# Sliding-window attention in periods of two groups: scores of both, turns and values interleaved anew, and VectorE's two code paths joined

## The chip, the cores and the metric

The kernel runs on one core of a Trainium2 chip. The metric is the device time of one execution in microseconds (us). Engines in the profile: PE is TensorE's matmuls and PEld its weight loads, DVE is VectorE, ACT is ScalarE, POOL is GpSimd, SP is SyncE, which here issues DMAs.

## What is computed

Three stages, one after the other: attention with a window and sinks (2 batches, 8 heads, 768 positions, head width 64), a gated two-layer network, and a dense mixture of four experts. Cut to what matters:

```python
# attention: q, k, v are (2, 8, 768, 64); n_sink = 4, window = 128
scores = matmul(q, k.T) / sqrt(64)
keep = (key < n_sink) | ((0 <= query - key) & (query - key < window))
a = softmax(where(keep, scores, -1e9))
x = matmul(a, v)                      # then (1536 tokens, 512)
# first network: w_in (512, 2048), w_out (2048, 512)
h = x @ w_in
x = (h * tanh(softplus(h))) @ w_out
# four experts: w1 (4, 512, 1024), w2 (4, 1024, 512)
out = sum(p[:, e] * (relu(x @ w1[e]) @ w2[e]) for e in range(4))
```

## The kernel before

**Units and groups.** Attention goes head pair by head pair: `CT` = 4 passes `ct`, of which pass 0 is written out and passes 1 to 3 are a loop on PE and DVE (ACT's and POOL's are written out). A pass has 24 units: 2 batches x 6 query tiles of 128 x 2 heads. Four units are a group, so a pass has 6 groups (`GROUPS_A`), 24 groups in all. A window of 128 lets a query tile see two key tiles and 16 sink columns, 272 columns. The first two tiles of a batch have 128 and 256 columns; so groups 0 and 3 of a pass are short, the others full. Four passes of six groups fill about the first 80 us.

**A group's way.** PE forms scores (`scores`, L650), one PSUM bank for each unit, four banks in all (`score_bank`): unit u goes to the bank of u-4 and waits for `masked`, the count of units that DVE has masked. DVE adds the mask and takes the row minimum in one custom instruction and a read of the accumulator (`mask_unit`, L1485), into one of four slots that ACT must have emptied. ACT takes the exponential (`exponent`, L1066) and sums the rows. DVE inverts the sums of a group (`invert`, L1495 and L1498), POOL multiplies (`normalise`, L479) and, in full groups, gathers the sink columns (L494). PE turns the group (`turn`, transposes L701, the sinks L704), in two halves; ACT copies the first half out (`copy_first`, L1077) and DVE the second (`copy_second`, L1533 for the sinks, L1537). PE multiplies with the values (`values`, L731, sinks L737). When a half of a batch is summed up, ACT takes `x_hi` (L1062) and DVE `x_lo` (L1505) from the bank (`take`).

**Order.** It is written out by hand for each engine; each engine runs its instructions in this order, and semaphores tie them together. A period handles one group g: on PE scores of g, values of g-3, turn of g-2 (`TURN_LAG`, `VALUES_LAG`); on DVE the second copy of g-3, two masks, the inverse of g-1, two masks, with a take before or behind; on ACT four exponentials with the first copy of g-2 among or behind them. Some periods of ACT also carry a weight split of 128x1024 (`SPLIT_AT`), some of POOL a DMA (`ADD_AT`). After the last group the first three up-projections of the network (`start_up`) lie between the last turns and values on PE.

**The first network** runs in 6 rounds `t` of 8 steps (`STEPS`). In each step s PE forms an up-projection (L635) and, three steps late (`LAG`), a down-projection (L838). Between them lies the gate: DVE `start_gate` (L1441), `gate_lo` of s-2 (L1479), `finish_first` (L1457, L1460), `square` (L1447), `finish_second` (L1467, L1473), with ACT's exponentials between. PE waits for `mish_lo`, which `gate_lo` counts. In the fourth step of a round DVE also adds up the last round (`add_up`, L1634).

**Two paths.** A flag computed from `n_sink` and `window` decides between the path for a window and a general path. The code of DVE was all in both paths: attention and all networks, `networks()`; the path for a window branches at its end over the other to the end of the program. The inputs here take the path for a window.

## Time and profile before

| | us |
|---|---|
| median of 3 runs | 853.79 |
| lowest, highest | 853.73, 853.82 |
| the profiled execution | 853.87 |
| its span, first to last instruction | 852.0 |
| PE busy in the span | 841.8 |
| DVE, ACT, POOL busy | 605.3, 401.5, 172.2 |

The span is one execution, taken by the hardware profiler; 1.9 us of its time lie around the span. Ends of matmuls are modelled and consecutive ones overlap in the records, so a PE that is busy in all its time can still have gaps between starts. The weight load that precedes each matmul has its own rows (PEld), and their starts show the rhythm better. A row of the timeline may stand for several equal instructions (x8); the number in brackets is the idle time of the engine before it and who ended it, or "issue" where nothing that the profile shows did.

### The profile page before, as it was taken

The page shows a single profiled execution, that of the slowest core. Times are in us where ns is not written, and L with a number is a line of the kernel's source. Part 1 is how long each engine was busy: PE and PEld are TensorE (multiplying, and loading weights), DVE is VectorE, ACT ScalarE, POOL GpSimd, SP SyncE. Part 2 cuts the span into 40 slices and gives each one's busy share as a digit, 9 for nine tenths or more (in the row PEclk, how much of TensorE's full clock was granted, in tenths as well). Part 3 has the DMA queues.
Part 4 walks back from the last instruction along what each step waited for, and adds up shares of the span by engine and source line. Part 5 has one row for each costly group of instructions (what it writes and reads, how often), then busy time and mean ns, then how long its engine had stood idle before and what let it go on. Part 6 is the DMA issues. An engine that isn't in the chain of part 4 may idle for free.

```text
span 852.0 us, 13889 instructions
## 1 busy us (share of the span) xinstructions
PE 841.8 (99%) x4518; PEld 729.0 (86%) x4518; DVE 605.3 (71%) x1170; ACT 401.5 (47%) x739; POOL 172.2 (20%) x259
## 2 busy tenths in 40 slices
PE   6999999999999999999999999999999999999998
PEld 5777888888888888898999899989998998899897
DVE  7888799898888989876565565565565655656655
ACT  6999754448754549753324314314413423432310
POOL 6778200001100112222012112102202202202100
PEclk9999999999999999999999999999999999999999
DMA  7455730004830006825145135225315415403304
GB/s 257 143 164 155 158 98 1 1 0 99 202 95 0 0 0 133 164 50 117 21 100 117 34 83 117 47 70 117 62 55 117 79 38 117 98 22 65 68 1 149
DMA packets 25621, 72.69 MB, mean 85 GB/s; under 512 B 4336, under 2 KB 6512, under 8 KB 25584
## 3 DMA queue, kind: packets, MB, share of 16 engines
q0 software_dynamic: 10720, 33.82, 21.9%
q1 hardware_dynamic: 14576, 38.04, 13.3%
q10 hardware_dynamic: 288, 0.39, 0.1%
q8 instruction: 16, 0.26, 0.1%
q14 instruction: 21, 0.17, 0.1%
HBM read 35.28 MB, written 3.15 MB: 45 GB/s over the span
## 4 chain that ended last, share of the span: by engine, by line
PE 99%; DMA 0%; POOL 0%; DVE 0%; issue 0%; SPq 0%; DVEq 0%
PE banks L943 31%; PE banks L869 28%; PE banks L838 15%; PE banks L635 15%; PE banks L650 3%; PE banks L731 3%; PE banks L701 3%; PE banks L737 1%; DMA pool<-kT 0%; POOL pool L479 0%; PE banks L704 0%; PE banks L956 0%; DVE pool L1485 0%; DVE pool L1842 0%; SPq L397 0%
## 5 line engine op out<-in xcount | busy, mean ns | idle before, releaser
L1767 DVE SCALAR_TENSOR_TENSOR pool<-banks,p_norm,pool 128x512 f32<-128x512 f32 x179 | 132.8, 748 | 66.1 <-PE banks L943 64.3
L943 PE MATMUL banks<-w_hi,g_lo 128*128 128x512 f32 x382 | 149.9, 392 | 0.0
L943 PE MATMUL banks<-w_lo,g_hi 128*128 128x512 f32 x382 | 149.7, 392 | 0.0
L943 PE MATMUL banks<-w_hi,g_hi 128*128 128x512 f32 x382 | 148.6, 389 | 0.0
L1290 ACT ACTIVATE g_hi<-pool 128x384 fp32r<-128x384 f32 x96 | 50.5, 526 | 190.7 <-DVE pool L1747 139.1
L869 PE MATMUL banks<-x_hi,w_lo 128*128 128x384 f32 x256 | 86.0, 336 | 0.0
L869 PE MATMUL banks<-x_hi,w_hi 128*128 128x384 f32 x256 | 85.9, 335 | 0.0
L869 PE MATMUL banks<-x_lo,w_hi 128*128 128x384 f32 x256 | 85.7, 335 | 0.0
L943 PEld LDWEIGHTS banks<-w_hi,g_lo 128*128 128x128 f32 x382 | 71.6, 188 | 15.0
L943 PEld LDWEIGHTS banks<-w_hi,g_hi 128*128 128x128 f32 x382 | 71.7, 188 | 13.8 <-issue 0.2
L943 PEld LDWEIGHTS banks<-w_lo,g_hi 128*128 128x128 f32 x382 | 71.7, 188 | 13.8
L547 POOL DMA_DIRECT2D w_lo<-w_sum x15 | 13.1, 876 | 322.9 <-ACT w_lo L1202 322.9
L1284 ACT ACTIVATE g_hi<-banks 128x384 fp32r<-128x384 f32 x32 | 15.7, 491 | 131.2 <-PE banks L869 131.2
L838 PE MATMUL banks<-g_hi,w_hi 128*128 128x512 f32 x192 | 75.1, 391 | 0.0
L635 PE MATMUL banks<-x_hi,w_hi 128*128 128x512 f32 (+1 forms) x192 | 75.1, 391 | 0.0
L838 PE MATMUL banks<-g_lo,w_hi 128*128 128x512 f32 x192 | 74.8, 390 | 0.0
L838 PE MATMUL banks<-g_hi,w_lo 128*128 128x512 f32 x192 | 74.8, 390 | 0.0
L635 PE MATMUL banks<-x_lo,w_hi 128*128 128x512 f32 (+1 forms) x192 | 74.7, 389 | 0.0
L635 PE MATMUL banks<-x_hi,w_lo 128*128 128x512 f32 (+1 forms) x192 | 74.7, 389 | 0.0
L1754 DVE SCALAR_TENSOR_TENSOR g_lo<-pool,g_hi 128x384 fp32r<-128x384 f32 x96 | 53.6, 559 | 21.6 <-ACT g_hi L1290 17.8
L1037 ACT ACTIVATE pool<-pool,two 128x512 f32<-128x512 f32 x48 | 34.8, 725 | 72.2 <-DVE pool L1447 72.2
L1725 DVE TENSOR_TENSOR pool<-banks,pool 128x384 f32<-128x384 f32 x32 | 17.8, 557 | 52.9 <-ACT pool L1221 44.5
(151 smaller groups left out, 1774.8 us busy)
## 6 DMA issues: line engine op xcount, KB each, us to landing
w_raw<-weights SPq DMA_DIRECT2D x48, 512.0 KB, 4.3
w_lo<-w_raw POOLq DMA_DIRECT2D x48, 512.0 KB, 5.5
w_lo<-w_sum POOLq DMA_DIRECT2D x15, 384.0 KB, 4.0
pool<-v SPq DMA_DIRECT2D x8, 384.0 KB, 3.3
out<-pool SPq DMA_DIRECT2D x11, 256.0 KB, 2.0
pool<-kT SPq DMA_DIRECT2D x7, 400.0 KB, 5.1
pool<-qT SPq DMA_DIRECT2D x7, 384.0 KB, 4.4
w_lo<-pool POOLq DMA_DIRECT2D x2, 384.0 KB, 4.8
```

Of the source, the lines that this page charges most:

```text
L635: mm = pe.matmul(banks[:, 4 + f % H_RING, :], w[:, f, k * P:(k + 1) * P], x[:, k, ds(c * CHUNK, CHUNK)], start=(k == 0 and n == 0), stop=( ...
L650: mm = pe.matmul(bank[:, col:col + n], q_pair[rows, b, j * P:(j + 1) * P], k_pair[rows, b, key:key + n], start=True, stop=True)
L701: mm = pe.transpose(banks[:, TURN_BANK + n, P * (2 * h + k):P * (2 * h + k) + P], window_prob(u + h, WIDE)[:, col:col + P], ident[:, :])
L731: mm = pe.matmul(banks[D * h:D * h + D, out_bank, column], v_pair[:, b, kt, D * h:D * h + D], prob_T[:, slot, P * (2 * h + k):P * (2 * h + ...
L838: mm = pe.matmul(banks[:, i, :], w[:, f, lo:hi], g_slot(h, g), start=(f == 0 and n == 0), stop=(f == STEPS - 1 and n == 2), skip_group_che ...
L869: mm = pe.matmul(banks[:, bank, 0:HALF], w_cols(w, p2 * SLOT + at + k * P, P), x_part(lo, s, name)[:, k * HALF:(k + 1) * HALF], start=(fir ...
L943: mm = pe.matmul(banks[:, bank, :], g[:, s, f * SUP + at:f * SUP + at + P], w_cols(w, p2 * SLOT + DOWN_AT[f], DM), start=(f == 0 and n == ...
L1037: act.activation(r_buf[:, s % 2, :], n_buf[:, s % 2, :], ACT.Ln, bias=two[:, 0:1]).then_inc(l_done, 1)
L1290: act.activation(relu_of(s, f, l), source, ACT.Relu).then_inc(relu_hi, 1)
L1725: dve.tensor_tensor(c12, bank(5 + s), p1_sum, ALU.add).then_inc(sum_done, 1)
L1754: dve.scalar_tensor_tensor(out=g_lo[:, s, at], in0=source, scalar=0.0, in1=g_hi[:, s, at].bitcast(f32), op0=ALU.max, op1=ALU.subtract).the ...
L1767: dve.scalar_tensor_tensor(out=to, in0=d_bank, scalar=share, in1=to, op0=ALU.mult, op1=ALU.add)\
```

## The change

On PE the period now handles two groups, g (even) and g+1: scores of g, scores of g+1, turn of g-2, values of g-3, values of g-2, turn of g-1. ACT copies the first half of g-2 behind the exponentials of g, and of g-1 behind those of g+1; its takes move accordingly. DVE's period of two groups opens as before with the second copy of g-3, then two masks, the inverse of g-1, two masks; then the take of g-4, three masks of g+1, the second copy of g-2, the inverse of g, the last mask, the take of g-3. The inverse and the copy of an even group thus come one period of a group earlier than before.

On DVE the functions of the networks move out of `networks()`. Each path runs attention and the first `OWN_ROUNDS` = 2 rounds of the first network and then branches to a common piece `dve_rounds`, which has the other four rounds and all that follows. The branch hint at DVE's end is gone. The arithmetic, the buffers, the semaphores and the DMAs are the same; POOL and SP have the same instructions.

```diff
+OWN_ROUNDS = 2
 # PE
                 def period(ct, g, before):
                     scores(ct, g)
+                    scores(ct, g + 1)
+                    even = group_at(ct, g, TURN_LAG, before)
+                    if even:
+                        turn(*even)
                     if at := group_at(ct, g, VALUES_LAG, before):
                         values(*at)
-                    if at := group_at(ct, g, TURN_LAG, before):
+                    if even:
+                        values(*even)
+                    if at := group_at(ct, g + 1, TURN_LAG, before):
                         turn(*at)
-                for g in range(GROUPS_A):
+                for g in range(0, GROUPS_A, 2):
                     period(0, g, False)
 # ACT
                 for ct in range(CT):
                     for g in range(GROUPS_A):
-                        for u in range(4 * g, 4 * g + 4):
...
-                            exponent(window_prob(u, w), scores_w[:, u % 4, 0:w], u % 4, u)
-                            if u % 4 == (1 if g % (QT // 2) == 0 or ct * GROUPS_A + g == 2 else 3):
-                                if at := group_at(ct, g, TURN_LAG, ct > 0):
-                                    copy_first(*at)
-                        if at := group_at(ct, g, VALUES_LAG, ct > 0):
-                            take_after(*at)
+                        copied = group_at(ct, g, TURN_LAG, ct > 0)
+                        if g % 2 == 0:
+                            exponents(ct, g, range(4))
+                            if copied:
+                                copy_first(*copied)
+                        else:
+                            exponents(ct, g, range(2))
+                            if at := group_at(ct, g, VALUES_LAG + 1, ct > 0):
+                                take_after(*at)
+                            exponents(ct, g, range(2, 4))
+                            if copied:
+                                copy_first(*copied)
+                            if at := group_at(ct, g, VALUES_LAG, ct > 0):
+                                take_after(*at)
 # DVE
                 def period(ct, g, before):
-                    copied = group_at(ct, g, TURN_LAG + 1, before)
-                    ended = group_at(ct, g, VALUES_LAG + 1, before)
-                    first_half = ended is not None and ended[1] % (QT // 2) == 1
-                    if copied:
-                        copy_second(*copied)
+                    if at := group_at(ct, g, TURN_LAG + 1, before):
+                        copy_second(*at)
                     mask_scores(ct, 4 * g)
                     mask_scores(ct, 4 * g + 1)
-                    if ended and not first_half:
-                        take_after(*ended)
                     if at := group_at(ct, g, 1, before):
                         invert(at[0], 4 * at[1], 4)
                     mask_scores(ct, 4 * g + 2)
                     mask_scores(ct, 4 * g + 3)
-                    if first_half:
-                        take_after(*ended)
+                    if at := group_at(ct, g, VALUES_LAG + 1, before):
+                        take_after(*at)
+                    for u in range(4 * g + 4, 4 * g + 7):
+                        mask_scores(ct, u)
+                    if at := group_at(ct, g, TURN_LAG, before):
+                        copy_second(*at)
+                    invert(ct, 4 * g, 4)
+                    mask_scores(ct, 4 * g + 7)
+                    if at := group_at(ct, g, VALUES_LAG, before):
+                        take_after(*at)
...
             with nc.body("dve_window", valid_engines=[mybir.EngineType.DVE]):
                 window_attention()
-                leaving = networks()
-                dve.br("dve_end").branch_hint(leaving)
+                rounds(0, OWN_ROUNDS)
+                dve.br("dve_rounds")
...
-            nc.switch_bb("dve_end")
+            nc.switch_bb("dve_rounds")
+            rounds(OWN_ROUNDS, NC * MISH)
```

Two places in the order of instructions. First PE in pass 0, from the scores of group 4 on. L650/L651 are scores, L701/L702 and L704/L705 turns, L731/L732 and L737/L738 values; the semaphores that an instruction waits for stand in brackets. Before:

```order
L650 MATMUL banks<-pool 128x272 [waits masked] x4
L731 MATMUL banks<-pool 64x128 [waits first_copied,masked,sink_out,sink_zero]
L731 MATMUL banks<-pool 64x128 x3
L737 MATMUL banks<-pool 64x128 x2
L731 MATMUL banks<-pool 64x128 [waits masked,second_copied]
L731 MATMUL banks<-pool 64x128 x3
L737 MATMUL banks<-pool 64x128 x2
L701 MATMUL banks<-ident,prob_third 128x128 [waits first_copied,prob_ready]
L701 MATMUL banks<-ident,prob_third 128x128 x3
```

And now, at the same place:

```order
L651 MATMUL banks<-pool 128x272 [waits masked] x8
L702 MATMUL banks<-ident,prob_third 128x128 [waits first_copied,prob_ready]
L702 MATMUL banks<-ident,prob_third 128x128 x3
L702 MATMUL banks<-ident,prob_third 128x128 [waits second_copied,prob_ready]
L702 MATMUL banks<-ident,prob_third 128x128 x2
L702 MATMUL banks<-ident,prob_third 128x128 [waits sink_out,sinks_ready]
L705 MATMUL banks<-ident,pool 64x128
L732 MATMUL banks<-pool 64x128 [waits first_copied,masked,sink_out,sink_zero]
L732 MATMUL banks<-pool 64x128 x3
L738 MATMUL banks<-pool 64x128 x2
```

Eight units' scores stand in a row where four stood, each waiting for a mask, and the turn of group 2 has moved ahead of the values of group 1.

Second, DVE in pass 0 from the second copy of group 1 on (L1553 the sinks, L1557 the rest) to the fourth mask of group 4; a mask is two rows of L1505, the inverse is L1515 and L1518. Now:

```order
L1553 COPY pool<-banks 64x128 [waits turned]
L1557 COPY pool<-banks 128x512
L1505 ISA pool,row_min<-banks,mask 128x272 [waits scored,exp_done]
L1505 ISA row_min 128x1
L1505 ISA pool,row_min<-banks,mask 128x272 [waits scored,exp_done]
L1505 ISA row_min 128x1
L1515 TENSOR_SCALAR row_den<-row_sum 128x4 [waits prob_ready,exp_done]
L1518 RECIPROCAL row_den<-row_den 128x4 [waits den_sum]
L1505 ISA pool,row_min<-banks,mask 128x272 [waits scored,exp_done]
L1505 ISA row_min 128x1
L1505 ISA pool,row_min<-banks,mask 128x272 [waits scored,exp_done]
L1505 ISA row_min 128x1
```

The twelve rows of before are the same but for the line numbers (L1533, L1537, L1485, L1495, L1498). Nothing moved here; what moved are PE's next scores, which now wait for these masks directly.

## Rows read from the trace of the kernel before

**Rows 1.** The page: busy time of each engine; PE and its clock in 40 slices.

```profile
PE 841.8 (99%) x4518; PEld 729.0 (86%) x4518; DVE 605.3 (71%) x1170; ACT 401.5 (47%) x739; POOL 172.2 (20%) x259
...
PE   6999999999999999999999999999999999999998
...
PEclk9999999999999999999999999999999999999999
```

**Rows 2.** About one attention pass: stretch, length, busy PE, PEld, DVE, ACT, POOL, clock.

```profile
35.00:55.00 20.00, 20.00 (x220) 15.47 (x220) 17.37 (x76) 18.50 (x62) 15.72 (x30) 1.00 0.56 156
```

**Rows 3.** PE's weight loads, three groups: start us, us, what, count, [idle before].

```profile
41.89 0.52 PEld L650 LDWEIGHTS banks<-pool 64*128 64x128 f32 x8 [0.17 <-issue]
42.75 0.63 PEld L731 LDWEIGHTS banks<-pool 128*64 128x64 f32 x12 [0.33 <-ACT pool L1077]
43.55 0.86 PEld L701 LDWEIGHTS banks<-ident,pool 128*128 128x128 f32 x8 [0.17 <-issue]
...
44.69 0.76 PEld L650 LDWEIGHTS banks<-pool 64*128 64x128 f32 x8 [0.20 <-DVE row_min L1485]
45.80 0.42 PEld L731 LDWEIGHTS banks<-pool 128*64 128x64 f32 x8 [0.36 <-issue]
...
47.27 0.85 PEld L701 LDWEIGHTS banks<-ident,prob_third 128*128 128x128 f32 x8 [0.17 <-issue]
...
48.40 0.76 PEld L650 LDWEIGHTS banks<-pool 64*128 64x128 f32 x8 [0.20 <-issue]
49.52 0.42 PEld L731 LDWEIGHTS banks<-pool 128*64 128x64 f32 x8 [0.36 <-issue]
...
50.98 0.64 PEld L701 LDWEIGHTS banks<-ident,pool 128*128 128x128 f32 x6 [0.17 <-issue]
51.78 0.52 PEld L650 LDWEIGHTS banks<-pool 64*128 64x128 f32 x8 [0.17 <-issue]
```

**Rows 4.** PE's weight loads at the first values behind an up-projection.

```profile
84.19 0.63 PEld L731 LDWEIGHTS banks<-pool 128*64 128x64 f32 x12 [0.35 <-issue]
```

**Rows 5.** DVE from the copy of a turned group to its fourth mask.

```profile
48.51 0.28 DVE L1533 COPY pool<-banks 64x128 f32<-64x128 f32 x1 [0.75 <-PE banks L704]
...
49.34 0.44 DVE L1485 CUSTOM_DVE_ANT_0 pool<-banks,mask 128x272 f32<-128x272 f32 x1
...
50.55 0.44 DVE L1485 CUSTOM_DVE_ANT_0 pool<-banks,mask 128x272 f32<-128x272 f32 x1
...
51.28 0.08 DVE L1485 DVE_READ_ACCUMULATOR2_ANT row_min<- 128x1 f32 x1
```

**Rows 6.** DVE in the same place, behind a short group.

```profile
51.92 0.68 DVE L1537 COPY pool<-banks 128x512 f32<-128x512 f32 x1
...
53.11 0.42 DVE L1505 TENSOR_TENSOR x_lo<-banks,x_hi 128x256 f32 x1
53.45 0.16 DVE L1495 TENSOR_SCALAR row_den<-row_sum 128x4 f32<-128x4 f32 x1
...
54.62 0.08 DVE L1485 DVE_READ_ACCUMULATOR2_ANT row_min<- 128x1 f32 x1
```

**Rows 7.** POOL, one full group.

```profile
50.53 2.44 POOL L479 TENSOR_TENSOR pool<-pool,row_den 128x272 f32<-128x272 f32 x4 [1.70 <-DVE row_den L1498]
```

**Rows 8.** The first pass: DVE's mask 11 is read; PE's scores of group 4 begin.

```profile
12.28 0.08 DVE L1485 DVE_READ_ACCUMULATOR2_ANT row_min<- 128x1 f32 x1
...
14.98 0.76 PEld L650 LDWEIGHTS banks<-pool 64*128 64x128 f32 x8 [0.20 <-issue]
```

**Rows 9.** Network, step 16: DVE's start_gate and g_lo; PE's next down-projection.

```profile
169.73 0.69 DVE L1441 TENSOR_SCALAR pool<-banks 128x512 f32<-128x512 f32 x1 [0.89 <-PE banks L635]
170.34 0.68 DVE L1479 TENSOR_TENSOR g_lo<-pool,g_hi 128x512 fp32r<-128x512 f32 x1
...
174.97 0.39 PE L838 MATMUL banks<-g_hi,w_hi 128*128 128x512 f32 x1
```

**Rows 10.** The view of DMA issues: KB each, us to landing.

```profile
prm<-params SPq DMA_DIRECT2D x1, 2.0 KB, 3.6
```

More of the change, by code:

```diff
@@ L1682, in networks, with rounds @@
+            def rounds(first, behind):
+                for t in range(first, behind):
                     for f in range(STEPS):
@@ L1757, in evict @@
-                def evict(it, s, e, first, k):
-                    dve.wait_ge(tile_done, SUP_TILES * it + k + 1)
-                    tile = TILE_ORDER[k]
-                    to, d_bank = out_acc(s, tile), banks[:, (2 * s + k) % 4, :]
-                    token = s * SUP_TILES + tile
-                    share = p_norm[:, ds(e, 1), token:token + 1].rearrange("p a n -> p (a n)")
-                    if first:
-                        dve.tensor_scalar(to, d_bank, share, None, ALU.mult).then_inc(evicted, 1)
-                    else:
-                        dve.scalar_tensor_tensor(out=to, in0=d_bank, scalar=share, in1=to, op0=ALU.mult, op1=ALU.add)\
-                           .then_inc(evicted, 1)
@@ new lines, in halves_used, with sum_16, sum_15 @@
+            def halves_used(it, n):
+                if not isinstance(it, int) or it >= 1:
+                    dve.wait_ge(relu_lo, 4 * it - 4 + n)
+            def sum_16(it, s):
+                halves_used(it, 3)
+                dve.wait_ge(prod_done, 7 * it + (3 if isinstance(it, int) and it == 0 else 2))
+                dve.wait_ge(p1_copied, it + 1)
+                dve.tensor_tensor(c12, bank(5 + s), p1_sum, ALU.add).then_inc(sum_done, 1)
+            def sum_15(it, s):
+                halves_used(it, 2)
+                if isinstance(it, int) and it == 0:
+                    dve.wait_ge(x_added[0]["T3"], 16)
+                dve.wait_ge(prod_done, 7 * it + (4 if isinstance(it, int) and it == 0 else 3))
+                dve.tensor_tensor(c22, bank(7), p1_sum, ALU.add).then_inc(sum_done, 1)
@@ new lines, in relu_rest, with evict @@
+            def relu_rest(it, s, n):
+                f, l, source = ((0, 0, bank(4)), (1, 1, c22), (0, 1, c12), (1, 0, c21))[n]
+                dve.wait_ge(relu_hi, 4 * it + n + 1)
+                at = slice(f * SUP + l * HALF, f * SUP + (l + 1) * HALF)
+                dve.scalar_tensor_tensor(out=g_lo[:, s, at], in0=source, scalar=0.0, in1=g_hi[:, s, at].bitcast(f32),
+                                         op0=ALU.max, op1=ALU.subtract).then_inc(relu_lo, 1)
+            def evict(it, s, e, first, k):
+                dve.wait_ge(tile_done, SUP_TILES * it + k + 1)
+                tile = TILE_ORDER[k]
+                to, d_bank = out_acc(s, tile), banks[:, (2 * s + k) % 4, :]
+                token = s * SUP_TILES + tile
+                share = p_norm[:, ds(e, 1), token:token + 1].rearrange("p a n -> p (a n)")
+                if first:
+                    dve.tensor_scalar(to, d_bank, share, None, ALU.mult).then_inc(evicted, 1)
+                else:
+                    dve.scalar_tensor_tensor(out=to, in0=d_bank, scalar=share, in1=to, op0=ALU.mult, op1=ALU.add)\
+                       .then_inc(evicted, 1)
@@ new lines, in _ @@
+            last = NC * MISH - 1
+            sum_16(0, 0)
+            difference(0, "T4")
+            gate_lo(NC * MISH * STEPS - 1)
+            sum_15(0, 0)
+            sum_22(0, 0)
+            sum_12(0, 0)
+            x_lo_of(0, "T4")
+            relu_rest(0, 0, 0)
+            relu_rest(0, 0, 1)
+            relu_rest(0, 0, 2)
+            dve.wait_ge(last_down, 1)
+            add_one(last, NC - 1, 0)
+            dve.wait_ge(last_down, 2)
+            add_one(last, NC - 1, 1)
+            dve.wait_ge(last_down, 3)
@@ new lines, in _ @@
+            add_one(last, NC - 1, 2)
+            dve.wait_ge(down_done, STEPS * (last + 1))
+            add_one(last, NC - 1, 3)
+            sum_21(0, 0)
+            x_lo_of(1, "B11")
+            relu_rest(0, 0, 3)
+            difference(1, "T1")
+            difference(1, "T2")
+            difference(1, "T3")
+            difference(1, "T4")
+            x_lo_of(1, "T2")
+            x_lo_of(1, "T1")
+            sum_16(1, 1)
+            x_lo_of(1, "T3")
+            sum_15(1, 1)
+            x_lo_of(1, "T4")
@@ new lines, in _ @@
+            pair_step(2 * PAIRS - 1, 1, E - 1, False)
+            for k in range(SUP_TILES - 1):
+                evict(2 * PAIRS - 1, 1, E - 1, False, k)
+            k, tile = SUP_TILES - 1, TILE_ORDER[SUP_TILES - 1]
+            for part in range(2):
+                dve.wait_ge(tile_done, SUP_TILES * (2 * PAIRS - 1) + k + part + 1)
+                to = out_acc(1, tile)[:, part * (DM // 2):(part + 1) * (DM // 2)]
+                dve.scalar_tensor_tensor(out=to, in0=banks[:, (2 + k + part) % 4, 0:DM // 2],
+                                         scalar=p_norm[:, E - 1, SUP_TILES + tile:SUP_TILES + tile + 1],
+                                         in1=to, op0=ALU.mult, op1=ALU.add).then_inc(evicted, 1)
```

260 lines of the change are left out of this document (99 added, 161 removed).

## The prediction

> **What bounds the kernel now.** I read the page first. TensorE (PE) is busy 841.8 of 852.0 us and granted full clock in all slices [rows 1]: whatever lengthens or shortens PE's own sequence moves the end by as much. In the attention stage (about 10 to 90 us) PE has no free time in the stretches of 20 us, while VectorE (DVE) has 17.37, ScalarE (ACT) 18.50 and GpSimd (POOL) 15.72 us of work in 20 [rows 2]. So I next took the timeline of PE's weight loads over three groups. It repeats with exactly 9.89 us per three groups (41.89 to 51.78), and gives each phase from start to start [rows 3]: scores (S) 0.86 us for a batch's first ("short") group and 1.12 for a full one; turns (T) 0.80 short, 1.13 full; values (V) 0.80 short, 1.46 full. In order: S .86, V .80, T 1.14, S 1.11, V 1.47, T 1.13, S 1.12, V 1.46, T .80.
>
> **What a switch costs.** A full V has 24 matmuls and takes 0.66 us more than a short one with 12, so 12 matmuls cost 0.66 and 0.14 us of the short phase is the change to the next kind of work. A full S streams 8 x 272 = 2176 columns, a short one 1536, for 0.26 us more: 0.41 ns a column, so 0.88 and 0.62 us of work and 0.24 us of switch. The loads of T are 0.11 us apart (0.86 for 8, 0.64 for 6): 0.66 of 0.80 is work, 0.14 switch. PE thus pays six switches in two groups, about 1.0 us.
>
> **Part 1, fewer switches (a gain).** Two groups now run S S T V V T. A switch after S (0.24) and one of 0.14 go away; what remains is S to T, T to V, V to T, T to S. S to T is costed like S to V (0.24, it ends the same matmuls), T to V like T to S (0.14 and up to 0.20). The trace has few of these two; the nearest worse row is the pause of 0.35 us before V after up-projections [rows 4], against 0.17 before T in the usual place. Upper bound: both 0.15 dearer. Gain taken: 0.38 us a pair, at least 0.1.
>
> In the Trainium skill, "TensorEngine Tiling (Array Packing)", section Key Properties, a change of tiling mode drains TensorE. The phases here do differ in tile shape, and the pauses agree; that page speaks for the change and has no word on what the new order waits for.
>
> **Part 2, a new wait (a loss).** Scores of unit u go to the bank that unit u-4 leaves, so they wait for the mask of u-4. Before, those masks belonged to the previous group and lay behind V and T. Now the scores of group g+1 follow at once on those of g and wait for the four masks of g. What stands ahead of these masks on DVE? Its period still opens with the second copy of the last turn, and that turn is still the last thing PE does before its scores. DVE's order up to the fourth mask is the same as now, and the trace shows how long it takes: PE starts scores at 48.40 [rows 3]; the copy starts at 48.51, the first mask at 49.34, the third (with the inverse of the sums ahead of it) at 50.55, and the last row minimum is read at 51.28 and lasts 0.08 [rows 5]. That is 2.96 us after PE's start, DVE without a pause. Adding 0.07 for the semaphore (ACT follows a mask by 0.1 us), the eighth unit's scores start 3.03 us into the period. Unhindered they would start after seven units' streaming. In pairs:
> - Groups 4,5 (both full): 2 x 0.88 less the last unit's 0.22, 1.54 us. Stall 3.03 - 1.54 = 1.49.
> - Groups 2,3 (full, short): 0.88 + 0.62 - 0.21 = 1.29. Stall 1.74.
> - Groups 0,1 (short, full): 0.62 + 0.66 = 1.28. Here the copy has no sinks and the masks are small. PE starts at 51.78, the fourth minimum is read at 54.62 plus 0.08, which is 2.92; a take of 0.34 (53.11 to 53.45) stands between and moves behind the masks, and 0.08 was a pause: 2.5, so the unit starts at 2.57 [rows 6]. Stall 1.29.
> Less 0.38 a pair, the three pairs are +1.11, +1.36 and +0.91: **+3.38 us for each pass over six groups**.
>
> Does anything else end later than PE in the stretched period? I laid one pair (4,5) out from PE's start. T of the even group starts at 3.03 + 0.22 + 0.24 = 3.49, its turn is out 1.24 later (4.7), the two copies on DVE take 0.9 (5.6). V of the odd group before it (1.32) runs from 4.6 to 5.9, then V of the even group, whose second half needs that copy only at 6.6: margin 1.0. In pair 0,1 the same margin is 0.2, the smallest. ACT's first copy waits for half the turn (4.2) and is done at 4.7. POOL needs 2.44 us for a group [rows 7]; the odd group's inverse is out at 2.15, so it is ready at 4.6 and turned at 7.4; the even group's starts at 6.0 and is needed in the next pair only, six us later. ACT's work is 18.5 in 20, or 6.1 us a pair with weight splits, under the new 7.4 to 8.2. So these cost nothing, covered by PE's own longer period; with that cover gone (were the stall not there) ACT would have only 0.1 us a pair to spare.
>
> **Part 3, the first pass.** Its scores for groups 0 to 3 now all come ahead of the first turn. The last of them waits for mask 11, whose minimum is read at 12.28 plus 0.08 [rows 8]. Then T(0) from 12.43 + 0.21 + 0.24 = 12.9, 0.80; its second copy (0.65) is out at about 14.4; V(0) 0.80, T(1) 1.13: scores of group 4 at about 16.4 instead of 14.98 [rows 8], +1.4. Pair 4,5 adds 1.11. The other pass bodies, three of them, add 3 x 3.38 = 10.1. The end (start-up of the network between the last turns) keeps its order.
>
> **Part 4, DVE's joined code.** DVE now jumps over the general path's code after round 1, between steps 15 and 16, at about 168.8 us. It waits 0.89 us for PE there anyway; the g_lo that follows it ends at 171.02 and PE uses it at 174.97 [rows 9], so another 3.9 us are free: 4.8 in all. Bounds: nothing, or one small transfer from memory, for which the 2 KB of parameters (3.6 us to landing) is the nearest [rows 10]. Either is hidden, and DVE regains 0.89 us a step. Taken: 0. The smaller program changes nothing that PE waits for.
>
> **The sum.** 1.4 + 1.1 + 10.1 = 12.6 us on the profiled execution's 853.87 (852.0 of span and 1.9 around it): 866.5, or **866.4 us** from the median 853.79. PE is full after attention, so nothing gives it back. The span should be 864.6.
>
> **The rivals.**
> - *The stall is hidden (the other side, faster).* If the masks of g were done before PE wants their banks, only the switches would remain: 11 pairs x 0.38 = 4.2 us, **849.6 us**. It decides when DVE's chain from the turn to the fourth mask is under 1.54 us. It is 2.96 by a row and has no pause in it. Only if DVE's copy came after the masks could this be; the order says otherwise. Chance 0.04.
> - *Dearer switches, or a second wait.* Both new switches at the upper bound add 0.3 us in each of 11 pairs, 3.3 in all; the small margin of pair 0,1 lost by 0.3 us adds 0.9 in three passes: **870.6 us**. The pause of 0.35 speaks for it, the pauses of 0.17 and 0.20 after T against it. Chance 0.12.
> - *Shorter stalls.* Masks on DVE that wait for nothing could move a little closer and the first pass may lose nothing: 1.4 less at the start and 0.2 less a pair, **862.8 us**. Chance 0.12.
> - *The jump of DVE.* If it took 3 us more than the 4.8 that are free, PE would stop for 3: **869.4 us**. Chance 0.03. The Trainium skill, "Runtime: NRT & Kernel Launch", section Instruction fetch mechanics, says that a taken branch out of the fetched pages stalls until its target page has been fetched. No row of this trace shows such a jump; by the page the jump costs something, and by rows it would have to cost more than 4.8 us to be seen.
> - *The change does nothing that shows:* gain and stall equal. This needs stalls of 0.4 us, a quarter of those worked out. Chance 0.02.
>
> **How the numbers follow.** The forecast's own case has 0.67. The range 861.5 to 871 takes in the rivals at 862.8, 869.4 and 870.6 and leaves out the two that end near or under the old time and what a lower granted clock would do (PE would be idle for a fifth of each pair; in the first slice of the page it is busy in only six tenths, and the granted clock is full there [rows 1], so I give that little). A measurement of this kernel can tell about 0.2% from no change. Faster 0.04, same 0.02, slower 0.94.
>
> **What would show it.** In the attention stage PE's busy share falls, with waits of S on DVE's row minimum (four units of each pair, about 1.4 us together); the pass takes 23.2 us instead of 19.8; PE's work is unchanged; the pause before V no longer stands after each S; behind attention every stretch is as long as before, shifted by 12.6 us. DVE's first instruction of step 16 may come late, with PE undisturbed. The prediction is wrong if S runs through without such waits, if PE waits on copies or POOL instead, or if the network stage gets longer.

## The result and the profile after

The changed kernel takes **867.96 us** (median; 867.81 to 869.23), the kernel before 853.82 beside it: 1.0169 times as long, 95% interval 1.0158 to 1.018. The profiled execution is itself at 867.96, 866.0 of it span. Its mean granted clock is 1.000, as in the other two of the five executions at the low end (867.81 and 867.85); the remaining two have 0.998 and took 868.77 and 869.23. The forecast was 866.4 us in 861.5 to 871.

The page of the kernel after: busy time of each engine, and PE and its clock in 40 slices.

```profile
PE 852.7 (98%) x4518; PEld 735.8 (85%) x4518; DVE 606.1 (70%) x1170; ACT 403.9 (47%) x739; POOL 172.0 (20%) x259
...
PE   7999999999999999999999999999999999999998
...
PEclk9999999999999999999999999999999999999999
```

Against [rows 1] the number of matmuls is the same, the clock is full in this execution, and only the first slices can tell anything. (PE's busy time grew by 10.9 us with the same work and the same clock. Its ends are modelled, so its share hides most of the waits; the starts of the weight loads are the better measure.) The windows of the attention stage are more distinct: stretch, length, then busy PE, PEld, DVE, ACT, POOL, and the clock.

```profile
35.00:55.00 20.00, 19.03 (x193) 14.60 (x195) 15.09 (x66) 16.21 (x54) 13.64 (x27) 1.00 0.54 154
```

In the same 20 us PE loaded weights 195 times where before it did so 220 times [rows 2], and every other engine did less too: the stage as a whole runs slower, no engine replaced PE as the one that is full. The view of waits names what PE waited for (us in total, times, longest):

```profile
PEld banks L651 <- DVE row_min L1505: 13.0, 21, 0.7
```

Before, the same wait was 1.2 us in six places of 0.2. Its place is in the timeline of PE's weight loads, here pair 4,5 of one pass: start us, us, what, count, [idle before].

```profile
40.21 0.76 PEld L651 LDWEIGHTS banks<-pool 64*128 64x128 f32 x8 [0.20 <-issue]
41.66 0.66 PEld L651 LDWEIGHTS banks<-pool 64*128 64x128 f32 x4 [0.69 <-DVE row_min L1505]
42.88 0.66 PEld L651 LDWEIGHTS banks<-pool 64*128 64x128 f32 x4 [0.56 <-DVE row_min L1505]
43.89 0.86 PEld L702 LDWEIGHTS banks<-ident,prob_third 128*128 128x128 f32 x8 [0.36 <-issue]
44.71 0.11 PEld L705 LDWEIGHTS banks<-ident,pool 128*64 128x64 f32 x1
45.02 0.42 PEld L732 LDWEIGHTS banks<-pool 128*64 128x64 f32 x8 [0.20 <-issue]
...
47.79 0.64 PEld L702 LDWEIGHTS banks<-ident,pool 128*128 128x128 f32 x6 [0.17 <-POOL pool L480]
48.60 0.52 PEld L651 LDWEIGHTS banks<-pool 64*128 64x128 f32 x8 [0.17 <-issue]
```

The first four units of scores run through, the next two pairs of units each wait for a row minimum, and turns begin 3.68 us after the scores (43.89 less 40.21). Nothing waits behind that: values follow the turn after 0.20, two groups of values run in one piece, the second turn follows after 0.17. DVE in the same stretch:

```profile
40.53 0.67 DVE L1557 COPY pool<-banks 128x512 f32<-128x512 f32 x1
41.16 0.44 DVE L1505 CUSTOM_DVE_ANT_0 pool<-banks,mask 128x272 f32<-128x272 f32 x1
41.53 0.08 DVE L1505 DVE_READ_ACCUMULATOR2_ANT row_min<- 128x1 f32 x1
...
41.89 0.17 DVE L1515 TENSOR_SCALAR row_den<-row_sum 128x4 f32<-128x4 f32 x1
...
42.37 0.44 DVE L1505 CUSTOM_DVE_ANT_0 pool<-banks,mask 128x272 f32<-128x272 f32 x1
...
43.10 0.08 DVE L1505 DVE_READ_ACCUMULATOR2_ANT row_min<- 128x1 f32 x1
```

This is the chain of [rows 5], now with PE at its end: the fourth minimum is read 2.97 us after PE began (43.10 + 0.08 less 40.21).

Starts of scores give the books of the stage. A pass over six groups lasts 19.8 us before and 23.94 after (24.66 to 48.60): pair 0,1 went from 6.51 to 7.85, pair 2,3 from 6.18 to 7.70, pair 4,5 from 7.09 to 8.39. The first pass body of the loop begins at 24.66 instead of 22.08, so the first pass lost 2.6 us. With 3 x 4.15 = 12.4 that is 15.0, and the first up-projection, the one behind the last scores, starts 15.0 us later (96.3 instead of 81.3). The network and the experts keep that distance to the last tile (861.8 instead of 846.7). Yet the span is only 14.0 us longer. One microsecond came back behind the last matmul.

### The profile page after: what moved, and what is told of

Same layout as the page of the kernel before. It is cut to its first block, busy times and chain, and to the rows that moved or that the text cites. A ratio compares the mean times of both kernels' runs of the same rounds, so it can differ in the third digit from the quotient of the medians.

```text
span 866.0 us, 13888 instructions
## 1 busy us (share of the span) xinstructions
PE 852.7 (98%) x4518; PEld 735.8 (85%) x4518; DVE 606.1 (70%) x1170; ACT 403.9 (47%) x739; POOL 172.0 (20%) x259
## 4 chain that ended last, share of the span: by engine, by line
PE 96%; DVE 1%; issue 1%; ACT 1%; DMA 0%; DVEq 0%; ACTq 0%
PE banks L951 30%; PE banks L877 27%; PE banks L846 15%; PE banks L636 15%; PE banks L702 3%; PE banks L651 2%; PE banks L732 2%; PE banks L738 1%; ACT pool L1074 1%; DVE pool L1557 0%; DMA prm<-params 0%; DVE row_min L1505 0%; PE banks L705 0%; PE banks L964 0%; DVE pool L1505 0%
```

## The experiments

### The two halves of the change

**e1**: only attention changed, in the code of before.

```diff
 def period(ct, g, before):
     scores(ct, g)
-    if at := group_at(ct, g, VALUES_LAG, before): values(*at)
-    if at := group_at(ct, g, TURN_LAG, before): turn(*at)
+    scores(ct, g + 1)
+    ... # turn(even), values(odd before), values(even), turn(odd), as in the change; ACT and DVE too
```

> Only the order of attention is changed, VectorE's two paths stay apart. Theory (the whole loss is the stall of the odd group's scores behind the even group's masks): 868 us, as the changed kernel, within 0.4. Rival (the joined code and its jump, before which the trace shows 2.27 us of idle VectorE instead of 0.89, carry part of the loss): 1.4 us less, 866.6.

Measured: 868.84 us (868.64 to 871.62), 1.0186 times before (1.0168 to 1.0203). Against the 853.86 us of before measured beside it, attention alone costs **15.0 us**, about 1 us more than the whole change. The longest of its four executions, 871.62 us, has a mean clock of 0.996; the three others have 1.000 and took 868.64 to 868.88.

**e2**: only DVE's code joined, attention in the old order.

```diff
 with nc.body("dve_window"):
     window_attention()
-    leaving = networks()
-    dve.br("dve_end").branch_hint(leaving)
+    rounds(0, OWN_ROUNDS)
+    dve.br("dve_rounds")
+# dve_rounds: rounds 2 and 3, the gate's end and the experts, once for both paths
```

> The opposite half: attention in the old order, VectorE's paths joined behind round 1. Theory: 853.8 us, no change, with a pause of about 2.3 us on VectorE ahead of step 16 and PE without a gap. Rival (the jump reaches PE): 855.2 or more, with a gap of PE in the down-projection some 5 us behind the jump.

Measured: 852.86 us (852.72 to 853.13 in ten runs), 0.9989 times before (0.9979 to 0.9998). The join is not free of effect: it **saves 1.0 us**, and makes this the fastest of all kernels here. The jump itself is in the timeline of DVE at step 16:

```profile
168.01 0.69 DVE L1474 SCALAR_TENSOR_TENSOR pool<-banks,pool 128x512 f32<-128x512 f32 x1
170.83 0.69 DVE L1442 TENSOR_SCALAR pool<-banks 128x512 f32<-128x512 f32 x1 [2.13 <-issue]
```

DVE has 2.13 us without work, against the 0.89 that it usually waits for PE [rows 9]; in the changed kernel the pause at the same step is 2.27. PE's row has no gap there in either kernel: the 4.8 us that were free cover it. By the Trainium skill, "Runtime: NRT & Kernel Launch", section Instruction fetch mechanics, a taken branch out of the fetched pages stalls until its target page is there. The trace agrees, and prices it here at 1.2 to 1.4 us more than the wait it replaces.

So where does the microsecond come from? The other jump. Before, DVE leaves the window path at the end of the program and jumps over the general path's code to the common end. The view of one source line (line, queue, operation, count, duration in ns, start) and that of waits, kernel before:

```profile
L116 SPq COMPARE_BRANCH  x1: 38/38/38, 851.3 to 851.3; - x1
...
L116 DVEq DRAIN  x1: 70/70/70, 851.7 to 851.7; - x1
...
SPq L116 <- DMA out<-pool: 2.1, 1, 2.1
```

and e2:

```profile
L117 DVEq DRAIN  x1: 524/524/524, 848.2 to 848.2; - x1
L117 SPq COMPARE_BRANCH  x1: 38/38/38, 850.5 to 850.5; - x1
...
SPq L117 <- DMA out<-pool: 1.4, 1, 1.4
```

DVE's last result is out at 848.82 before and at 848.68 in e2. Before, DVE reaches its closing drain 2.9 us later, at 851.7, behind even SP's wait for the last output; in e2 it is there at once. SP's wait for the last transfer ends 2.5 us after DVE's last result before, and 1.8 in e2; from that to the end of the span it is 0.7 against 0.4. Together 1.0 us. The second part ends with DVE's late drain. That the first, a slower last transfer, has to do with the fetching of DVE's code beside it is an inference; what the runs show is that the two go together (also in e1, with the jump: 2.5 and 3.2 us from the last result to SP's branch and to the end; and in e3, e4, e6 and e9, without it, DVE's drain starts with its last result and the end comes 2.1 to 2.2 us behind it).

### DVE's order inside the chain

**e3**: the inverse of the sums behind the four masks instead of between them.

```diff
     mask_scores(ct, 4 * g + 1)
-    if at := group_at(ct, g, 1, before): invert(at[0], 4 * at[1], 4)
     mask_scores(ct, 4 * g + 2)
     mask_scores(ct, 4 * g + 3)
+    if at := group_at(ct, g, 1, before): invert(at[0], 4 * at[1], 4)
```

> The changed kernel, but VectorE inverts the sums of the group before behind the fourth mask instead of between the second and third. It takes 0.48 us of the chain from the turn to the fourth mask. Theory (this chain paces PE): 11 pairs x 0.48 = 5.3 us less, 862.7 us, PE's wait ahead of the seventh unit's scores shorter by as much. Rival (PE is paced by what GpSimd normalises, which now starts 0.75 us later): no gain or slower, 868 to 870.

Measured: 862.68 us (862.47 to 862.82), 1.0103 times before (1.0086 to 1.012): 5.3 us less than the changed kernel. PE's loads in pair 4,5, the same place as above, and the view of waits:

```profile
38.23 0.76 PEld L651 LDWEIGHTS banks<-pool 64*128 64x128 f32 x8 [0.20 <-issue]
39.69 1.38 PEld L651 LDWEIGHTS banks<-pool 64*128 64x128 f32 x8 [0.69 <-DVE row_min L1505]
41.42 0.86 PEld L702 LDWEIGHTS banks<-ident,prob_third 128*128 128x128 f32 x8 [0.36 <-issue]
...
46.13 0.52 PEld L651 LDWEIGHTS banks<-pool 64*128 64x128 f32 x8 [0.17 <-issue]
...
PEld banks L651 <- DVE row_min L1505: 7.3, 13, 0.7
```

The second wait (0.56) is gone, the first stands as it was. Turns begin 3.19 us after the scores instead of 3.68: 0.49, the two instructions of the inverse. The pass is 22.54 us (23.59 to 46.13), 1.40 less, and the first pass gives the rest: the loop begins at 23.59 instead of 24.66.

**e4**: the copy of the turned probabilities behind the four masks too, the longest thing ahead of them.

```diff
-    if at := group_at(ct, g, TURN_LAG + 1, before): copy_second(*at)
     mask_scores(ct, 4 * g) ... mask_scores(ct, 4 * g + 3)
+    if at := group_at(ct, g, TURN_LAG + 1, before): copy_second(*at)
+    if at := group_at(ct, g, 1, before): invert(at[0], 4 * at[1], 4)
```

> The changed kernel, but VectorE makes the four masks of the even group first and the copy of the last turn and the inverse behind them. The masks can start 0.4 us after PE's first scores, so the fourth is read at 0.4 + 4 x 0.36 + 0.1 = 1.9 us instead of 2.96. Theory: 11 pairs x 1.05 = 11.6 us less, 856.4 us, a little above the kernel before. Rival (a second wait: PE's values wait for the copy, which is now out 2.8 us into the period): less than half of that gain, 862 or more.

Measured: 864.98 us (864.82 to 865.09), 1.013 times before (1.0113 to 1.0147). This was the miss that taught most. The time lies where the rival put it (862 or more), but the theory's first half failed too, not only its overlap: the kernel is slower than e3, and nothing of the copy's 0.9 us came back in the stall. DVE's first masks of pair 4,5, PE's loads around them, and one wait from the view of waits:

```profile
40.10 0.44 DVE L1505 CUSTOM_DVE_ANT_0 pool<-banks,mask 128x272 f32<-128x272 f32 x1 [1.56 <-PE banks L651]
...
37.43 0.42 PEld L732 LDWEIGHTS banks<-pool 128*64 128x64 f32 x8 [0.60 <-DVE pool L1557]
...
39.15 0.76 PEld L651 LDWEIGHTS banks<-pool 64*128 64x128 f32 x8 [0.20 <-issue]
40.60 1.38 PEld L651 LDWEIGHTS banks<-pool 64*128 64x128 f32 x8 [0.69 <-DVE row_min L1505]
...
PEld banks L732 <- DVE pool L1557: 1.7, 4, 0.6
```

DVE now stands idle for 1.56 us with the mask at the head of its queue, and still starts it 0.95 us after PE's first score (40.10 less 39.15). With the copy ahead it was also 0.95 (41.16 less 40.21). So the first score of a full group needs 0.95 us from the start of its loads until DVE begins on it, and the copy had been lying inside that time at no cost. Put behind the masks it only comes late for the values, in pair 2,3 of each looped pass (0.60, 0.37 and 0.37 us). The passes are 0.89, 0.69 and 0.69 us longer than e3's, 2.3 in all; what those waits leave of it was not taken apart.

**e7**: the other direction, one more piece of DVE's work (a take of 0.68 us) ahead of the four masks.

```diff
     if at := group_at(ct, g, TURN_LAG + 1, before): copy_second(*at)
+    if at := group_at(ct, g, VALUES_LAG + 1, before): take_after(*at)
     mask_scores(ct, 4 * g)
     ...
-    if at := group_at(ct, g, VALUES_LAG + 1, before): take_after(*at)
```

> The changed kernel, but VectorE's take of group g-4 stands ahead of the four masks instead of behind them: 0.61 us more in the chain in pair 2,3 and 0.34 us in pair 0,1 of each looped pass, none in pair 4,5. Theory (any work ahead of the fourth mask lengthens PE's period one for one): 3 x 0.95 = 2.9 us more, 870.9. Rival (the wait is set by when scores arrive, and VectorE has room): no change, 868.0.

Measured: 871.8 and 872.0 in two executions, 876.0 in two others, 1.0227 times before (1.0202 to 1.0252). The granted clock is 0.998 over the first two and 0.992 over the others; the four microseconds between them I put down to the clock, though only an execution of the longer kind was profiled. In it all of the lowered clock lies in the attention stage. Pair 2,3 in two passes: stretch, length, busy PE, PEld, DVE, ACT, POOL, clock.

```profile
61.00:65.00 4.00, 2.83 (x20) 1.87 (x19) 3.09 (x12) 2.38 (x7) 1.33 (x4) 1.00 0.00 0
65.00:71.00 6.00, 6.00 (x51) 5.09 (x52) 3.02 (x14) 4.35 (x15) 4.65 (x9) 0.72 0.04 5
...
91.00:96.00 5.00, 4.86 (x54) 4.01 (x55) 3.29 (x16) 4.49 (x17) 4.07 (x8) 1.00 0.12 10
```

The take makes the first wait of this pair 1.24 us instead of 0.69. In the undisturbed pass the pair takes 8.36 us instead of 7.70, as the theory of DVE's chain has it (0.61). In pair 0,1 the theory fails: 0.34 were expected, and the pair takes 7.93 us instead of 7.84, only 0.09 more. There the take delays the first mask by 0.27 (1.04 us after PE's start instead of 0.77) and the fourth by 0.09 (2.83 instead of 2.74). So not any work ahead of the fourth mask lengthens the period one for one. An estimate from these two pairs is 867.96 + 3 x 0.75 = 870.2 us at full clock; no execution of e7 had that. In the pass before it PE was busy 2.83 of 4 us, and then the granted clock fell from 2.4 GHz: it averages 0.72 over the next 6 us, a mixture of the two levels, and the same pair took 9.99. The profiled execution of the changed kernel does not pay this second cost (its clock is full in every slice). Its two executions at 0.998, 0.8 to 1.4 us longer than the three at 1.000, and the one of e1 at 0.996, 2.7 us or more longer than the rest of e1, may pay it; they were not profiled, so that is not shown.

### Is it DVE's work or the way there and back?

**e5** and **e6**: both attention orders with DVE nearly empty. Masks cover 16 columns instead of 272, the second copies are left out, and the arrays are filled once at the start; e5 does it in the kernel before, e6 in the changed one.

```diff
-    w = attention_plan(True)[0][j]
+    w = SINKS
...
-    dve.tensor_copy(sink_T[0:4 * SINKS, g % 2, :], sink_bank).then_inc(sink_out, 1)
+    dve.sem_inc(sink_out, 1)
...
-    dve.tensor_copy(*two_units).then_inc(second_copied, 1)
+    dve.sem_inc(second_copied, 1)
```

> The kernel before, with VectorE's part of attention made small: it masks and reduces 16 columns of each unit instead of 128 to 272, and leaves out the second copies of the turned groups (values are multiplied with what was there), so its output is not the reference's. It is the base for e6_light_after. Every theory: PE is full there anyway, so 853 to 855 us, a little for three added fills at the start.

Measured: 854.92 us, 1.0013 times before (1.0003 to 1.0022). Its pass is 19.8 us like before's; the first looped pass starts 1.0 us late (23.12 instead of 22.08), with the filling of the arrays ahead of it. PE's sequence bounds the old order even with this little work on DVE.

> The changed kernel with the same small VectorE work as e5_light_before (16 columns masked, no second copies; not the reference's output). Only the order of PE and ScalarE and the joined code differ from it. If stalls came from the length of VectorE's work alone, they are gone and two fewer switches a pair remain: 11 x 0.38 = 4.2 us less than e5, and 1.0 for the joined code, 5.2 in all. Rival, from the trace of e4_copy_behind (the first mask starts 0.95 us after PE's first scores though nothing is ahead of it): the fifth unit's scores, due at 0.88, still wait to about 1.2, a gap of 0.2 to 0.3 us a pair and PE's weight load uncovered behind it, so attention gains 0 to 1.5 us only, 1 to 2.5 us with the joined code.

Measured: 866.45 us (866.17 to 866.92), 1.015 times before (1.0133 to 1.0167). Both figures were missed. With hardly any work on DVE the new order, with the joined code, still costs 11.5 us over e5. Pair 4,5, first DVE, then PE's loads, kernel e6:

```profile
42.27 0.17 DVE L1511 CUSTOM_DVE_ANT_0 pool<-banks,mask 128x16 f32<-128x16 f32 x1 [1.57 <-PE banks L652]
...
42.61 0.17 DVE L1511 CUSTOM_DVE_ANT_0 pool<-banks,mask 128x16 f32<-128x16 f32 x1
...
43.25 0.17 DVE L1511 CUSTOM_DVE_ANT_0 pool<-banks,mask 128x16 f32<-128x16 f32 x1
...
41.33 0.76 PEld L652 LDWEIGHTS banks<-pool 64*128 64x128 f32 x8 [0.20 <-issue]
42.51 0.63 PEld L652 LDWEIGHTS banks<-pool 64*128 64x128 f32 x4 [0.42 <-DVE row_min L1511]
43.49 0.64 PEld L652 LDWEIGHTS banks<-pool 64*128 64x128 f32 x4 [0.35 <-DVE row_min L1511]
```

A mask of 16 columns is 0.17 us long instead of 0.44, but the first still begins 0.94 after PE's scores, and the second 0.34 behind it, where full masks are 0.36 apart. So a mask that is 0.27 us shorter shortens the chain by that once, at its last mask, and by 0.02 at each of the others; between light masks DVE stands still. Even the inverse is partly hidden there: it holds the third mask back by 0.30 us (0.64 between the second and the third), where with full masks it is 0.48. In pair 0,1 it is alike at another value, 0.77 us from the loads of a short score to its mask, in e9 (46.44 less 45.67) as in the changed kernel (49.37 less 48.60).

**e9**: e6 with the inverse behind the masks (the edit of e3).

> The kernel with the small DVE work in attention (masks of 16 columns, no second copies; what that leaves out is as in the run it is built on) and the inverse behind the four masks. The run it is built on took 866.45, with PE's second wait of a pair at 0.35 us and the first at 0.42 (pair 2,3). Latency theory: the first wait is the way of a score to its mask and back (0.94 us) and stays at 0.42; the second is made by the inverse, which holds the third mask back from 42.95 to 43.25, and goes to under 0.1. That is 0.28 to 0.35 us a pair, ten pairs (three passes of three and the one at the start): 2.8 to 3.5 less, 863.0 to 863.7. Rival, that the inverse was worth to the full kernel what it is worth here, one mechanism of DVE's queue: as with full masks, 5.3 us less, 861.2. Rival that a pair is set by PE's own pace and the inverse is in nobody's way when DVE is light: within 0.5 us of 866.45.

Measured: 860.3 us (860.2 to 860.82), 1.0079 times before (1.0062 to 1.0096): 6.15 less than e6, where 2.8 to 3.5 were expected and the one-mechanism rival had 5.3. PE's loads in pair 4,5:

```profile
38.12 0.76 PEld L652 LDWEIGHTS banks<-pool 64*128 64x128 f32 x8 [0.20 <-issue]
39.30 1.30 PEld L652 LDWEIGHTS banks<-pool 64*128 64x128 f32 x8 [0.42 <-DVE row_min L1511]
40.96 0.86 PEld L703 LDWEIGHTS banks<-ident,prob_third 128*128 128x128 f32 x8 [0.36 <-issue]
```

The first wait is 0.42 as before, the second is gone: the mechanism is the expected one. The size was not. In the first looped pass pair 4,5 gained the expected 0.31 and pair 0,1 0.40, but pair 2,3 gained 0.68. In e6 the fourth mask of that pair came 0.52 us late for a slot that ACT's exponentials free, and the first row below shows it. The others are the windows of e6's first pass (stretch, length, busy PE, PEld, DVE, ACT, POOL, clock):

```profile
36.41 0.17 DVE L1511 CUSTOM_DVE_ANT_0 pool<-banks,mask 128x16 f32<-128x16 f32 x1 [0.52 <-ACT prob_third L1076]
...
12.00:16.00 4.00, 2.98 (x18) 2.11 (x18) 1.66 (x13) 2.62 (x10) 3.66 (x7) 0.80 1.11 355
16.00:20.00 4.00, 4.00 (x30) 2.98 (x27) 0.93 (x9) 2.47 (x10) 2.67 (x5) 0.78 0.54 181
```

The first looped pass is 1.39 us shorter. In the two others e6 has only 0.28 of that wait for a slot, pair 2,3 gains 0.44, and the pass is 1.18 shorter: 3.75 in three, a little more than was expected. The other 2.1 us went before the loop, where e6 has a wait of 1.21 us for a mask and e9 two of 0.26 and 0.40. In that stretch of the profiled execution of e6 the granted clock is also 0.80 and 0.78, where e9's is full. The clock doesn't settle it, though: two other executions of e6 have a mean clock of 1.000 and took 866.38 and 866.53 us, no less than the profiled 866.17. How these 2 us divide stays open.

The lengths of the first and the second looped pass, each the distance of two starts of short groups' scores, give the ledger:

| kernel | first looped pass, us | second | second over before |
|---|---|---|---|
| before; e5 | 19.8; 19.8 | 19.78; 19.78 | |
| after | 23.94 | 23.92 | 4.1 |
| e3, inverse behind | 22.54 | 22.54 | 2.8 |
| e4, copy and inverse behind | 23.43 | 23.23 | 3.5 |
| e6, light | 22.98 | 22.76 | 3.0 |
| e9, light and inverse behind | 21.59 | 21.58 | 1.8 |

In the second pass moving the inverse is worth 1.38 us with full masks and 1.18 with light ones; the size of DVE's work is worth 1.16 with the inverse between the masks and 0.96 with it behind them. The two nearly add up over a pass, but not pair by pair: in pair 4,5 the inverse is worth 0.49 with full masks and 0.31 with light ones, and e6's wait for a slot in pair 2,3 makes up for part of the difference. (In the first pass, where that wait is longer, the sums agree even to 1.40 and 1.39, by coincidence.) What remains, 1.8 of 4.1 us, is neither. In pair 4,5 of e9 it can be added up: the last unit starts 2.19 us after PE's first score (40.25, the end of the fourth minimum, plus 0.06, less 38.12) instead of the unhindered 1.54 of the prediction, turns follow it 0.19 later than they would, and 0.38 of switches are saved; that makes 0.46, and the pair takes 7.55 us instead of 7.09. Scores that don't need a bank of the same pair might take that away too; that was not tried.

### The jump placed elsewhere

**e8**: before, with DVE's two paths swapped in memory, to see the join's gain by another route: no jump over general code at the end, nothing shared.

```diff
-with nc.body("dve_window"):
-    window_attention()
-    leaving = networks()
-    dve.br("dve_end").branch_hint(leaving)
 with nc.body("dve_general"):
     ...
+    networks()
+    dve.br("dve_end")
+with nc.body("dve_window"):
+    window_attention()
     networks()
     dve.br("dve_end")
```

> The kernel before with VectorE's two paths in the other order: the general path's code first, the path for a window last, nothing shared. VectorE then jumps over the general code at the start and falls through at the end. Theory (the 1.0 us that e2_join_only gained is the jump at VectorE's end, whose last instruction came 3.3 us behind its branch and the output's landing late by 0.7 us): the stretch from VectorE's last eviction to the end shrinks from 3.9 to 2.9 us, and the jump at the start, 1.3 to 2.3 us long and uncovered, delays attention by as much: 854.2 to 855.2 in all. Rival (the gain comes of the shorter code): the end keeps its 3.9 us, 855.2 to 856.2.

Measured: 865.1 us (864.8 to 865.99), 1.0133 times before (1.0116 to 1.015). Both figures were missed, since the jump at the start is dear: the first looped pass begins at 34.48 us instead of 22.08. DVE's first work behind it, and PE's:

```profile
13.91 0.44 DVE L1485 CUSTOM_DVE_ANT_0 pool<-banks,mask 128x272 f32<-128x272 f32 x1 [6.27 <-issue]
...
19.15 0.44 DVE L1485 CUSTOM_DVE_ANT_0 pool<-banks,mask 128x272 f32<-128x272 f32 x1 [4.79 <-issue]
...
20.79 0.29 PEld L701 LDWEIGHTS banks<-ident,pool 128*128 128x128 f32 x2 [11.25 <-POOL pool L479]
```

DVE stands for 6.27 us, does one mask, and stands for 4.79 more, while the DMA engines are full with the first loads; PE waits 11.25 us. That both pauses belong to the jump is an inference from their place. PE's clock falls within its pause and is still at half, its lower level of 1.2 GHz, when it works again, so part of the delay is the clock's (stretch, length, busy times, clock):

```profile
5.00:15.00 10.00, 4.94 (x24) 3.48 (x24) 2.53 (x16) 2.57 (x10) 2.87 (x4) 0.89 1.03 389
15.00:21.00 6.00, 0.21 (x1) 0.21 (x2) 1.72 (x9) 1.16 (x6) 1.02 (x3) 0.50 0.59 152
21.00:26.00 5.00, 4.55 (x26) 2.87 (x25) 4.10 (x21) 3.76 (x16) 4.60 (x9) 0.50 0.00 0
```

The end of the same kernel does what the join's did: DVE's last result is out at 861.23, its drain starts with it, and the span ends 2.2 us later instead of 3.2. So the gain of 1.0 belongs to the missing jump at the end, not to the sharing. (The branch hint went with the jump in e2 and in e8, and no run keeps one without the other.) The expectation had this part right: the end shrank by 1.0, though from 3.7 to 2.7 us behind the start of DVE's last instruction and not from 3.9 to 2.9. In these kernels the far jump was paid at the start and at the end of the program; only in the middle was it covered.

## Why the prediction was right, and where it was not

The time (867.96 for 866.4) and the sign came out, and the main mechanism, scores that wait for masks of their own pair. Two things in it were luck: the chain's length was right for a partly wrong reason, and two misses of opposite sign, in attention and at the end, took away part of each other. By its steps:

- **What bounds the kernel.** Right. Everything behind attention moved as one block, by 15.0 us, and nothing gave it back. ACT and POOL stayed covered: no long wait of PE names them.
- **Switches (Part 1).** Half right. T to V is 0.20 and two values run on without a break, as taken. The step left out what follows a starved unit: turns begin 0.65 us after the last unit's start and not 0.46 (0.22 + 0.24). That is 0.19 in pairs 0,1 and 4,5 and 0.16 in pair 2,3, and the 0.65 stands in e3 and e9 too. That the unit's weight loads could not run ahead under other matmuls is the likely reason; no run tests it. And the prediction's remark that the pauses agree with a drain at a change of tile shape does not hold: L702 to L705 changes from `128*128` to `128*64` without a pause (44.71), and L705 to L732 keeps `128*64` and has 0.20 (45.02). What a switch waits for stays open.
- **The stall (Part 2).** The chain of four masks was forecast at 3.03 us from PE's start, and the last unit of pair 4,5 did start there: the fourth minimum is out at 2.97, and PE's seventh unit begins 0.06 after the third minimum (42.88 for 42.82). In pair 2,3 likewise. In pair 0,1 the term was mis-sized: the chain took 2.74 us and not 2.5, because the masks there follow each other less closely than in the kernel before. The second begins 0.40 behind the first instead of 0.31, and the third, which waits 0.16 us for PE's own score, 0.34 behind the reciprocal's start instead of 0.28; with 0.03 at the first mask that is 0.18 of the 0.24. Pair by pair the cost was forecast at 0.91, 1.36 and 1.11 and measured at 1.34, 1.52 and 1.30. That is 0.77 too little a pass, 2.3 us in three; with 0.1 in the first pass that is all that attention was mis-sized by (15.0 against 12.6).
- **The reason for the stall.** The text took the chain for DVE's work, "without a pause". e4, e6 and e9 show it otherwise for full groups in the loop: 0.95 us from score to mask, then masks 0.36 apart at 272 columns and 0.34 at 16, with the inverse's 0.48 between them. (0.95 + 4 x 0.36 + 0.48 + 0.08 = 2.95; measured 2.97.) The sum was the same because the copy happened to fill the 0.95: luck. As an account of what to repair it was wrong: e3's gain was forecast to the tenth, e4's was off by more than 8 us.
- **The first pass (Part 3).** Scores of group 4 were forecast at 16.4 and start at 16.36; with pair 4,5 the forecast was 2.5 and 2.6 was measured.
- **DVE's jump (Part 4).** The jump is hidden, as taken. "The smaller program changes nothing that PE waits for" is true and beside the point: the end of the span waits for more than PE. The step missed the jump that the change takes away at the end of the program, 1.0 us. The prediction says that no row of the trace of before shows such a jump; the late drain at 851.7 was one.
- **The rivals.** The stall was not hidden; its condition, a chain under 1.54 us, is not met even with DVE nearly empty: in e9 the last unit still starts 2.19 us after the first. The shorter stalls did not come. Of the dearer switches up to 0.19 a pair did, in another place than named. The clock, to which little was given, stayed full in the profiled execution and in two more; the two executions at 0.998 are the longest of the five. In e7, with 0.55 us more of stall in pair 2,3, the mean was 0.998 or 0.992 in each of the four.

So the forecast was 1.6 us low, of which 1.4 are explained: attention was put 2.4 too low and the end 1.0 too high.

## What to carry to other kernels

Before two batches of matmuls are put side by side to save switches, count the accumulator banks: if the second needs the banks of the first, PE waits for the whole way out and back, and a leaner consumer shortened that here by no more than about a quarter (0.96 to 1.16 of 4.1 us a pass). In this chain, what lay inside the latency was free (the copy) and what lay between two links was paid in full (the inverse, 0.49), so look which rows are idle before you move work out. And when an engine's code gets a new layout, price every jump that it adds and every one that it removes, the last of the program too.

The Trainium skill, "Perfetto Trace Analysis", section Matmuls, advises to rotate independent groups of matmuls through different banks, so that the emptying of one overlaps the next group. The runs agree with that and add the size: here eight units in four banks cost 0.6 us a pair, switches saved already taken off, even with the lightest masks (1.8 a pass, e9).

## What the runs showed of the hardware that was not expected

- DVE begins on the first score of a full group 0.94 to 0.95 us after the start of that score's loads, with full masks or light ones, with the copy ahead or without; of a short group 0.77 us after. In the loop masks follow each other by 0.36 us at 272 columns and by 0.34 at 16; in e9's first pass, which is written out, those of 16 are only 0.26 apart (17.70 to 17.96).
- A jump of DVE to code far away cost 1.2 to 1.4 us more than the wait it replaced in the middle of the program, and 2.9 us until the closing drain at its end (1.0 us of it in the span). At the start, beside the first loads at 389 GB/s, DVE stood 6.27 and then 4.79 us.
- In e8 the clock fell within a pause of 11.25 us of PE, and stayed at 1.2 GHz while PE was busy 4.55 of 5 us. In e7 it fell after a stretch in which PE was still busy 2.83 of 4 us. The mean clock differed between executions of the same kernel (0.998 and 0.992 in e7, 1.000 and 0.998 in the changed kernel).
